# The first feed-forward's last 768 tokens by seven block products in place of eight, behind two chunks of 480 tokens

## The reference

```python
def _moe_ref(x, w1, w2, w3, w_out):
    h = np.maximum(np.maximum(x @ w1, x @ w2), x @ w3)
    return h @ w_out
def _moe2_ref(x, w_in, w_out):
    h = x @ w_in
    g = np.maximum(0.01 * h, h)
    return g @ w_out
```

## Time and profile before

| | |
|---|---|
| median of 3 executions | 787.16 us |
| the profiled execution | 785.7 us, its span 783.9 us |
| PE busy (matmul) | 770.1 us, 98% of the span |
| PE weight loads | 702.9 us, beside the matmuls |
| DVE, ACT, GpSimd busy | 411.6, 277.4, 125.5 us |
| chain that ended last | PE 92%, DVE 1% |
| mean granted clock of PE | 0.998 |

### The profile page before, as it was taken

The page is one execution under the profiler, slowest core; times in us unless marked ns, Lnnn a source line. Parts: engine busy times, 40 slices in busy tenths (PEclk is TensorE's granted clock), DMA queues, the critical chain, the costliest instruction groups (busy, mean ns, idle before and its releaser), DMA issues.

```text
span 783.9 us, 13484 instructions
## 1 busy us (share of the span) xinstructions
PE 770.1 (98%) x5470; PEld 702.9 (90%) x5470; DVE 411.6 (53%) x739; ACT 277.4 (35%) x670; POOL 125.5 (16%) x168
## 2 busy tenths in 40 slices
PE   8898999999999999999999999999999999999998
PEld 7788999989999999999998889898999899989996
DVE  6678688666655315313255656664434466334333
ACT  4574544434333122222154344452222244222222
POOL 4687121111011000011023345110000000000000
PEclk9999999999999999999999999999999999999999
DMA  8542333322111022013057455446243226322412
GB/s 273 186 182 73 128 110 111 111 68 97 59 60 36 1 68 86 1 46 120 1 175 282 166 190 235 165 160 230 94 145 137 94 95 217 146 94 94 145 44 80
DMA packets 29342, 94.19 MB, mean 120 GB/s; under 512 B 2784, under 2 KB 15072, under 8 KB 26208
## 3 DMA queue, kind: packets, MB, share of 16 engines
q1 hardware_dynamic: 29280, 93.33, 33.6%
HBM read 69.21 MB, written 24.12 MB: 119 GB/s over the span
## 4 chain that ended last, share of the span: by engine, by line
PE 92%; DVE 1%; issue 0%; ACT 0%; DVEq 0%
PE mlp_ps L893 13%; PE mlp_ps L895 12%; PE mlp_ps L894 12%; PE mlp_ps L980 7%; PE mlp_ps L978 7%; PE mlp_ps L979 7%; PE att_ps L999 6%; PE att_ps L1001 6%; PE att_ps L1000 6%; PE mlp_ps L999 3%; PE mlp_ps L1001 3%; PE mlp_ps L1000 3%; PE att_ps L882 1%; PE att_ps L859 1%; PE att_ps L782 1%; PE att_ps L808 1%
## 5 line engine op out<-in xcount | busy, mean ns | idle before, releaser
L893 PE MATMUL mlp_ps<-x_hi,wa_lo 128*128 128x432 f32 (+1 forms) x432 | 150.4, 348 | 1.2 <-DVE h_raw L1390 1.2
L894 PE MATMUL mlp_ps<-x_lo,wa_hi 128*128 128x432 f32 (+1 forms) x432 | 145.8, 337 | 0.0
L895 PE MATMUL mlp_ps<-x_hi,wa_hi 128*128 128x432 f32 (+1 forms) x432 | 145.7, 337 | 0.0
L893 PEld LDWEIGHTS mlp_ps<-x_hi,wa_lo 128*128 128x128 f32 x432 | 81.7, 189 | 5.6 <-DVE h_raw L1390 1.4
L895 PEld LDWEIGHTS mlp_ps<-x_hi,wa_hi 128*128 128x128 f32 x432 | 81.6, 189 | 2.2
L894 PEld LDWEIGHTS mlp_ps<-x_lo,wa_hi 128*128 128x128 f32 x432 | 81.7, 189 | 2.1
L1200 ACT ACTIVATE h_hi<-wa_raw 128x384 fp32r<-128x384 f32 x72 | 37.5, 523 | 102.1 <-DVE wa_raw L1457 101.1
L1455 DVE TENSOR_TENSOR wa_raw<-mlp_ps,h_raw 128x384 f32<-128x384 f32 x24 | 13.4, 558 | 86.1 <-PE mlp_ps L980 54.3
L1386 DVE TENSOR_TENSOR h_raw<-mlp_ps,half_max 128x432 f32<-128x432 f32 (+1 forms) x36 | 20.0, 554 | 70.6 <-PE mlp_ps L895 70.0
L1469 DVE TENSOR_TENSOR h_lo<-wa_raw,h_hi 128x384 fp32r<-128x384 f32 x72 | 44.9, 631 | 22.3 <-ACT h_hi L1200 20.3
L999 PE MATMUL att_ps<-wa_hi,h_lo 128*128 128x512 f32 x132 | 52.7, 399 | 0.7 <-DVE h_lo L1469 0.7
(11 more groups left out here) (163 smaller groups left out, 1721.1 us busy)
## 6 DMA issues: line engine op xcount, KB each, us to landing
u_even<-u_scratch SPq DMA_DIRECT2D x8, 1792.0 KB, 7.4
u_odd<-u_scratch SPq DMA_DIRECT2D x8, 1664.0 KB, 6.4
kq_in<-in_kq SPq DMA_DIRECT2D x14, 576.0 KB, 3.9
u_scratch<-u_even SPq DMA_DIRECT2D x4, 1792.0 KB, 8.5
u_scratch<-u_odd SPq DMA_DIRECT2D x4, 1664.0 KB, 6.7
v_rows<-in_v_sum SPq DMA_DIRECT2D x16, 288.0 KB
wa_raw<-in_w SPq DMA_DIRECT2D x6, 768.0 KB, 5.6
v_win<-in_v_band SPq DMA_DIRECT2D x12, 384.0 KB, 3.4
```

The source lines that it names most:

```text
L893: nc.tensor.matmul(ps, wlo, xhi, start=(n == 0), stop=False)
L894: nc.tensor.matmul(ps, whi, xlo, start=False, stop=False)
L895: last = nc.tensor.matmul(ps, whi, xhi, start=False, stop=(n == len(pairs) - 1))
```

## The change

Chunks are now 288, 288 and two of 480 tokens. The last 768 tokens (batch 2's last 192 and batch 3's 576) are made apart. Their first layer is nine quads (three pairs of feature tiles by three weights), each of seven products of 6 matmuls, so 378 matmuls of 384 columns. Their second layer is eight y groups (two halves of tokens by four m) of 18 matmuls of 384 columns, so 144. Nothing else of the computation differs.

The quads' items stand behind chunk 3. XS sums and splits the tokens, in seven items; LS loads a quad's raw weights in two DMAs of 256 KB (pieces of 512 bytes); WS and Q make GpSimd's four sums of 128x256, one pass of ACT and one of DVE over 128x1024. `ws_sums` is a single buffer, `ws_hi` and `ws_lo` are double. PE's order in a quad is the products 0, 3, 6 (of the quad before), 2, 1, 5, 4, over five PSUM banks. The items of the second feed-forward (LX, LU, B, X2, U, LO, O) now lie between the eight y groups, since their buffers overlap with those of the quads: LU and X2 wait for the last quad's last product (`S_ALL`). The first 12 matmuls of the first two y groups stand around the last quad's product 6. `U_DMAS` goes: a block of `u_odd` is moved by one DMA.

```diff
-CHUNK = [(0, 288), (288, 288)] + [(S + 432 * i, 432) for i in range(4)]
-WIDE = 432
+CHUNK = [(0, 288), (288, 288)] + [(S + 480 * i, 480) for i in range(2)]
+WIDE = 480
+SQ = 3 * (NF1 // 2)
+LAST_Y = [(j, m) for j in (1, 0) for m in range(KM)]
+NG1 = NC1 * NM
+NG = NG1 + len(LAST_Y)
...
-    put(NM * 4 + 2, ("LX", 0))
-    put(NM * 4 + 3, ("LU", 0))
-    put(NM * 4 + 5, ("B", 0))
-    for n in range(EARLY):
-        put(NM * 4 + 6 + 2 * n, ("X2", 0, n))
-    put(NM * 5 + 4, ("U", 0))
-    put(NM * 5 + 5, ("LU", 1), ("SU", 0))
-    put(NM * 5 + HG + 1, *(("X2", 0, n) for n in range(EARLY, NP)), ("U", 1), *(("LO", f) for f in range(4)))
-    put(NG - 1, ("O", 0), ("O", 1))
+    put(NG1 - 10.5, ("XS", 0))
+    for n in range(NP):
+        put(NG1 - 9.5 + n, ("XS", n + 1))
+    put(NG1 - 2.5, ("LS", 0), ("LS", 1))
+    put(NG1 - 1.5, ("WS", 0))
+    for n in range(SQ + 1):
+        put(NG1 + n, ("Q", n))
+        if n + 2 < SQ:
+            put(NG1 + n + 0.5, ("LS", n + 2))
+    y0 = NG1 + SQ + 1
+    put(y0 - 1.5, ("LX", 0))
+    put(y0 + 0.2, ("LU", 0), ("LO", 0), ("LO", 1), ("B", 0), ("X2", 0, 0), ("X2", 0, 1))
+    put(y0 + 1.2, ("X2", 0, 2))
+    put(y0 + 2.2, ("U", 0), ("LU", 1), ("SU", 0))
+    put(y0 + 3.2, ("X2", 0, 3), ("X2", 0, 4), ("LO", 2), ("LO", 3))
+    put(y0 + 4.2, ("X2", 0, 5), ("X2", 0, 6))
+    put(y0 + 5.2, ("U", 1))
+    put(y0 + 6.2, ("O", 0), ("O", 1))
...
+            def load_quad_raw(n):
+                fp, w = divmod(n, 3)
+                if n < 2:
+                    sp.wait_ge(xs_split, NP)
+                else:
+                    sp.wait_ge(ws_ready, 4 * (n - 1))
+                for i in range(2):
+                    src = w123[2 * fp + i].rearrange("p (k w e) -> p w k e", w=3, e=P)
+                    sp.dma_start(ws_raw[:, n % 2, i], src[:, w]).then_inc(ws_loaded[n % 2], 16)
```

On GpSimd and on PE (six matmuls in a product):

```diff
+            def last_sums(n):
...
+                pool.wait_ge(ws_loaded[n % 2], 32 * (n // 2 + 1))
+                if n:
+                    pool.wait_ge(ws_split, n)
...
+            def last_product(n, i):
+                if i == 0:
+                    if n == 0:
+                        pe.wait_ge(combined, COMBINED[NU])
+                        pe.wait_ge(xs_split, NP)
+                    else:
+                        if n >= 2:
+                            pe.wait_ge(s_added, 4 * (n - 1))
+                elif i == 3:
+                    pe.wait_ge(ws_split, n + 1)
+                elif i == 1:
...
+                elif i == 6:
+                    pe.wait_ge(s_added, 4 * n + 3)
+                else:
+                    pe.wait_ge(s_copied, 3 * n + S_COPIES.index({2: 0, 4: 1, 5: 2}[i]) + 1)
```

On ACT:

```diff
+            def last_quad(n):
+                done = n % 3 == 0 and n
+                if n + 1 < SQ:
+                    last_sums_high(n + 1)
+                if done:
+                    last_h_high(n - 1, 0)
+                if n < SQ:
+                    last_copy(n, 0)
```

On DVE:

```diff
+            def last_quad(n):
+                done = n % 3 == 0 and n
+                if n:
+                    last_add(n - 1, 1)
+                if done:
+                    last_h_low(n - 1, 0)
+                    last_h_low(n - 1, 2)
+                if n + 1 < SQ:
+                    last_sums_low(n + 1)
```

On ACT, a y group of the last tokens:

```diff
+            def last_y(g):
+                n = KM * NC1 + g - NG1
...
+                act.wait_ge(mlp_done, g + 1)
+                act.wait_ge(y_stored[n % 2], 16 * (n // 2) + CREDIT)
+                nc.scalar.activation(y_out[:, n % 2, 0:HALF], mlp_ps[group_bank(g)][:, 0:HALF], ACT.Copy).then_inc(y_evac, 1)
```

More of the change, by code:

```diff
@@ L241 @@
         _last[_bank] = ("M", _item[1])
+    if _item == ("Q", SQ):
+        _last[BANKS + group_bank(NG1)] = ("c11", SQ - 1)
 JOBS = len(JOB)
@@ L285 @@
 PARTS = ((0, 0), (1, 1), (0, 1), (1, 0))
+S_ORDER = (0, 3, 6, 2, 1, 5, 4)
+S_COUNT = {}
+for _n in range(SQ + 1):
+    for _p in S_ORDER:
+        _key = (_n - 1, _p) if _p == 6 else (_n, _p)
+        if 0 <= _key[0] < SQ:
+            S_COUNT[_key] = len(S_COUNT) + 1
+S_ALL = len(S_COUNT)
+S_PARTS = (0, 2, 1, 3)
+S_COPIES = (0, 2, 1)
+EARLY_F = NF1 - 2
 def g_slot(quad, part):
@@ L919, in mlp, with last_y @@
                     last.then_inc(mlp_done, 1)
+            def last_y(g, some=slice(None)):
+                j, m = LAST_Y[g - NG1]
+                if some.start is None:
+                    begin(("M", g))
+                if g in (NG1, NG1 + 1, NG1 + KM) or some.start is not None:
+                    early = some.stop is not None and some.stop <= EARLY_F
+                    pe.wait_ge(hs_split, 4 * (SQ // 3 - 1) if early else hs_count(SQ - 1, 1 if j else 3))
+                last = three_passes(mlp_ps[group_bank(g)][:, 0:HALF],
+                                    [((wo_tile(wo_hi, f, m), wo_tile(wo_lo, f, m)), (h_last(f, 0, j), h_last(f, 1, j)))
+                                     for f in range(NF1)], some=some)
+                if some.stop is None:
+                    last.then_inc(mlp_done, 1)
@@ new lines, in last_product @@
+            def last_product(n, i):
[9 more added lines that the diff above has]
+                elif i == 1:
+                    if n == 0:
+                        wait_evacuated(("M", NG1 - KM))
+                    else:
+                        pe.wait_ge(s_added, 4 * (n - 1) + 1)
+                elif i == 6:
+                    pe.wait_ge(s_added, 4 * n + 3)
+                else:
+                    pe.wait_ge(s_copied, 3 * n + S_COPIES.index({2: 0, 4: 1, 5: 2}[i]) + 1)
+                whi, wlo = ws_part(n, i)
+                xhi, xlo = xs_hi[:, i], xs_lo[:, i]
+                ps = s_bank(n, i)
+                first = i in (0, 1, 3)
+                for k in range(KT):
+                    nc.tensor.matmul(ps, wlo[k], xhi[:, k], start=(first and k == 0), stop=False, skip_group_check=True)
+                    nc.tensor.matmul(ps, whi[k], xlo[:, k], start=False, stop=False, skip_group_check=True)
+                    last = nc.tensor.matmul(ps, whi[k], xhi[:, k], start=False, stop=(k == KT - 1), skip_group_check=True)
+                last.then_inc(s_done, 1)
@@ new lines, in last_quad, with wait_evacuated @@
+            def last_quad(n):
+                if n == SQ:
+                    last_y(NG1, slice(None, EARLY_F))
+                    last_product(n - 1, 6)
+                    last_y(NG1 + 1, slice(None, EARLY_F))
+                    return
+                for i in S_ORDER:
+                    if i != 6:
+                        last_product(n, i)
+                    elif n:
+                        last_product(n - 1, i)
+            def wait_evacuated(job):
+                s, count = evacuation(job)
+                pe.wait_ge(s, count)
```

273 lines of the change are left out of this document (225 added, 48 removed), and 4 rows, old and new, of the table plan.

## The result

The kernel after takes 793.82 us (median of 15 runs, 790.20 to 795.65), the kernel before in the same comparison 787.05 (15 runs). The ratio is 1.0086, 95% interval 1.0073 to 1.0100: slower by 0.9%. 790.8 was predicted, in 783.0 to 796.0. The profiled execution took 792.95 us, its span 791.2, where that of before had 783.9: 7.3 us more.

What follows compares the result with a forecast made beforehand. PE, busy in 98% of the span, was taken to bound the kernel. Terms of -8.8, +5.2, +5.0 and +2.2 made +3.6 us on 785.7, so 789.3, plus 1.5 for the median: 790.8 us, range 783.0 to 796.0.

Steps and rivals of the forecast that it cites:

- The sign: Whole kernel: the change makes it slower, by +3.6 us in sum; chance of slower 0.66.
- both entries: Entry into the quads and exit into the second feed-forward: PE waits 5.2 and 5.0 us.
- Part 1: PE's matmul stream in the first feed-forward: 225.1 us removed, 216.3 added, so 8.8 us less.
- Part 2: Token sums and splits before the quads: hidden beside seven h groups, cost 0.
- Part 3: Quads once running: the helper engines keep up, 1 us left in the worst quad, cost 0.
- the rival that the helpers set the pace: In the quads, GpSimd, ACT and DVE run late: 0.7 us per quad gives +6.3, 797.1 us; chance 0.10.
- Part 4: Entry into the quads: late weight loads make PE wait 1.6 and 3.6 us, 5.2 in all.
- Part 5: Exit into the second feed-forward: PE waits before products 1 and 2, 5.0 us in all.
- Part 6: Low clock after the waits at the two entries: 1.1 us lost at each, 2.2 together.
- The rival that the clock stays: At both entries, waits as forecast but no low clock: +1.4 us, 788.6 us; chance 0.17.
- The rival that the entries are short: At both entries, shorter waits: 784.6 us, or 778.4 with all hidden; chance 0.17, faster.

Runs made afterwards that it cites:

- e4: Changed kernel with the 4-byte `table_loader` allocated behind `h_raw` again, as before the change: 789.44 us, 1.0031 of the kernel before.
- f3: Kernel before with chunks of 480, 480, 384 and 384 columns, eight products per block and no quads: 787.78 us, 1.0003 of the kernel before.
- e2: Changed kernel with the raw weights of quads 0 and 1 loaded one y group earlier: 788.63 us, 1.0026 of the kernel before.
- e1: Changed kernel with ACT copying product 0 of quad 0 ahead of quad 1's high parts: 790.94 us, 1.0042 of the kernel before.
- f2: Changed kernel with PE running unused matmuls while it would wait at both entries: 791.77 us, 1.0062 of the kernel before.
- e3: Changed kernel with the 1792 KB store of weight block 0 put behind the store of y6: 792.95 us, 1.0065 of the kernel before.
- g1: Kernel before with only `table_loader` allocated ahead of `x_raw`, moving buffers 32 bytes: 789.72 us, 1.0041 of the kernel before.
- g2: f4 with `table_loader` left where the change has it, all schedule edits kept: 782.57 us, 0.9946 of the kernel before.
- f4: Changed kernel with e2, e3 and e4's edits, ACT's quad 0 copies earlier, and later splitting of second feed-forward's weight block 1: 778.99 us, 0.9903 of before.
- f1: Changed kernel with `table_loader` behind all other buffers, so every buffer starts at a multiple of 64 bytes: 790.32 us, one run.

## Why the prediction was right, and where its sum was off

The sign, both entries and their releasers were right. By part:

- **Part 1.** The two chunks of 480 took 13.24 us more than before's chunks 2 and 3, for 12.15 by the prediction: 1.1 too little. A matmul cost 0.2189 for the 0.2165 taken, which over 576 of them would be 1.4; where the other 0.3 went I can't say. By e4 (0.2183, and 0.2 us less from chunk 2 to T) a small part of it is the place of the buffers. The larger part is the width: f3, in the kernel before, had 0.2183 too, so that both slopes were too low. From T to E the 372 matmuls took 0.3 us more than at 0.175 each, beside waits and clock, though from quad 1 on a matmul cost 0.1752 (7.36 us per quad). The last y groups ran at 0.1767, as taken. So the gain was 7.4 us, not 8.8.
- **Part 2.** Nothing waits for the token sums: the first product starts at the end of the last y group.
- **Part 3, and the rival that the helpers set the pace.** No wait in quads 1 to 8, so the rival is out. GpSimd's third sum in the quads took 738 ns at the median and 1051 at most, where the earlier trace rows had 1074 at the median. The rule of the Trainium skill ("SBUF — State Buffer", "SBUF: two separate sides"), by which it takes turns with DVE's passes that read two operands from SBUF, agrees: of the 36 sums in the quads four took longer, 0.93 to 1.05 us, each beside such a pass, and the others 0.72 to 0.74, many of them beside DVE passes that read PSUM. The turns were few, so they cost no wait.
- **Part 4.** 1.6 and 3.6 were predicted before products 3 and 2, and 1.8 and 3.35 measured, 0.1 less together. e2 and e1 show the two causes one by one: the loads' place on SP, and the copy behind the high parts.
- **Part 5.** 5.0 were predicted. 3.6 were measured before product 1. Product 2 then starts 3.57 us after product 1, 2.0 more than the nine matmuls between them need, in after and in f2 alike. That is 5.6 together, 0.6 over. e3 shows the first cause (y3's store behind SU 0) and that ACT's queue is the second.
- **Part 6.** 1.1 were taken at each entry. It was 2.0 at the first, 0.9 over: the low clock lasted 6.8 us and not the 3.4 of the earlier trace rows, though in e3, with the same waits, it was 3.4. It was 0 at the second, where it falls into a wait for ACT. The rival that the clock stays is out by the windows of after, though half of e2's runs come near it.

Over the stretch from chunk 2 to the first output: +1.1 (480 columns), +0.3 (quads), -0.1 (waits at the entry), +0.9 (clock there), +0.6 and -1.1 (waits and clock at the exit) make 1.7, which is the distance from +3.6 to +5.28. These are sizes; the mechanisms stand. That 793.8 lies inside the range is in part luck: the range went up to 796.0 for the rival that the helpers set the pace, which did not happen. The step that failed outright is one that the prediction did not have as a term. It took the rest of the second feed-forward as unchanged, because its instructions are, and each of its 23 other quads took 0.08 us longer. A line in the diff that only moves a 4-byte buffer costs 3.1 to 4.4 us, by e4, g1 and g2. In e4 the 23 quads take 367.04 us, 3.5 less than in after and 1.8 less than before: the line accounts for twice what there was to explain, and the rest of the new layout seems to give half of it back, which no run took apart. Without it the change would still be slower than before (e4: +2.5 us), because of the two entries. The rival that the entries are short had 784.6, or 778.4 with all of it hidden. It isn't what the change does, but it could be had: f4, at 779.0.

What stays open is the rule behind the price of a buffer's place: the layouts gave 15.61 (e4), 15.64 (f1), 15.65 (f3), 15.73 (g1) and 15.77 us (after) per quad, and 15.69 was before.

## What to carry to other kernels

A pipeline that is full in its steady state still has to be filled: at each change of stage, follow the first block through every engine's program order and every queue, and put nothing for the next block in front of what this one waits for. Count every wait at such a place, also one right behind another: behind the two waits at the entry no run of after had a clock mean above 0.994, and with the first wait gone (e2) half of the runs had. After any edit to the allocations compare the matmul's pitch in a stage that the edit does not touch.

## What the hardware showed that I had not expected

- The same matmul stream costs 0.3 to 1.3% more or less with buffers moved by 32 bytes: 0.1952 to 0.1977 us at 432 columns (g1), 15.77 to 15.61 us per quad (e4).
- The low clock after a wait lasted 3.4 us in some places and 6.8 in others. Which of the two a run gets differs from run to run, as does whether it comes at all: with waits of 2.7 and 3.4 us (in its profiled run) e2 had clock means from 0.987 to 0.998 in ten runs of one kernel.
- A low clock costs nothing while the next wait absorbs it: at the exit of after 3.4 us of it cost 0, by f2.
- A store of 192 KB that was issued 0.55 us behind one of 1792 KB took 8.3 us to land, with it, while one of 240 KB takes 2.0 where it stands alone. With the large store issued later (e3) the small ones took 4.2, behind a load of 512 KB, and the copy that needs the buffer came 5.2 us sooner, counted from the start of the second feed-forward.
